# Attention units interleaved with an expert layer: transposes and outputs of a unit moved three and four places behind the next unit's scores

## The reference, cut to what matters

```python
# q, k, v: 4 batches x 8 heads x 576 positions x 64
q_d, k_d, v_d = (a.reshape(B, H, 144, 4, D).mean(axis=3) for a in (q, k, v))
out_up = np.repeat(softmax_attention(q_d, k_d, v_d), 4, axis=2)          # "down" part, 144 x 144
scores = np.where(abs(pos[:, None] - pos[None, :]) < 4, scale * q @ k.T, -1e9)
out_local = softmax(scores) @ v                                           # "local" part, a band of 7
x = (out_up + out_local).transpose(0, 2, 1, 3).reshape(2304, 512)
x = (silu(x @ w_gate) * (x @ w_val)) @ w_out                              # first layer, hidden 1536
h = x @ w_in                                                              # second layer, hidden 2048
out = (maximum(h, 0) + alpha * minimum(h, 0)) @ moe2_w_out
```

## The kernel before, in words

| after its scores | PE | ACT | DVE |
|---|---|---|---|
| 0 | scores, L933 and L923 | | mask, maxima, shift (L730 to L747) |
| 1 | | exponentials (L545, L538) | |
| 2 | | | sums and reciprocals (L753 to L760), after which POOL normalises (L484, L487) |
| 3 | | | average of v (L719) |
| 4 | | | flip of the local part (L768) |
| 5 | transposes of the down part (L964) | turn (L556, four copies), then copy of the transposes (L566) | average of the next unit's q and k (L708) |
| 7 | outputs, L980 and L993 | | `add_up` (L776, L779) |
| 8 | | `x_hi` (L570) | `x_lo` (L785) |

## Time and profile before

### The profile page before, as it was taken

The page is one execution under the profiler, slowest core; times in us unless marked ns, Lnnn a source line. Parts: engine busy times, 40 slices in busy tenths (PEclk is TensorE's granted clock), DMA queues, the critical chain, the costliest instruction groups (busy, mean ns, idle before and its releaser), DMA issues.

```text
span 958.6 us, 21368 instructions
## 1 busy us (share of the span) xinstructions
PE 938.9 (98%) x8808; PEld 883.4 (92%) x8808; DVE 520.7 (54%) x1072; ACT 290.7 (30%) x759; POOL 143.1 (15%) x166
## 2 busy tenths in 40 slices
PE   5999999999999999999999999999999999999998
PEld 3899999999999999999999999999999999999997
DVE  8787655656655656556543545444444444444443
ACT  5665332423334333323333522111111111111111
POOL 7875000000010010100005830000000000000000
PEclk7899999999999999999999999999999999999999
DMA  9752211312222213113006520010100100200000
GB/s 285 238 175 81 87 54 49 96 49 62 85 59 78 68 54 92 54 49 94 25 11 198 168 92 1 1 66 1 35 32 1 67 1 1 67 1 1 34 1 34
DMA packets 32142, 63.37 MB, mean 66 GB/s; under 512 B 3376, under 2 KB 14640, under 8 KB 32048
## 3 DMA queue, kind: packets, MB, share of 16 engines
q1 hardware_dynamic: 32048, 62.02, 20.5%
HBM read 52.57 MB, written 9.44 MB: 65 GB/s over the span
## 4 chain that ended last, share of the span: by engine, by line
PE 95%; DVE 2%; POOL 1%; issue 1%; ACT 1%; DMA 0%; DVEq 0%; SPq 0%
PE ps L1031 52%; PE ps L1076 21%; PE ps L1059 16%; PE ps L980 2%; PE ps L923 2%; PE ps L933 1%; POOL w_lo L468 1%; PE ps L993 1%; PE ps L964 1%; DMA qk<-qk 0%; PE ps L1040 0%; ACT turned_early L556 0%; POOL down_one L487 0%; DVE qk_d_early L708 0%; ACT down_one L538 0%
## 5 line engine op out<-in xcount | busy, mean ns | idle before, releaser
L1031 PE MATMUL ps<-x_hi,w_hi 128*128 128x288 f32 x765 | 231.6, 303 | 0.0
L1031 PE MATMUL ps<-x_lo,w_hi 128*128 128x288 f32 x765 | 225.8, 295 | 0.0
L1031 PE MATMUL ps<-x_hi,w_lo 128*128 128x288 f32 x765 | 225.2, 294 | 0.0
L626 ACT CAST h_hi<-hidden 128x288 fp32r<-128x288 f32 (+1 forms) x192 | 90.9, 473 | 397.5 <-DVE hidden L894 330.9
L862 DVE TENSOR_TENSOR h_lo<-hidden,h_hi 128x288 fp32r<-128x288 f32 (+1 forms) x192 | 114.5, 596 | 84.7 <-ACT h_hi L626 82.2
L1031 PEld LDWEIGHTS ps<-x_hi,w_hi 128*128 128x128 f32 x765 | 143.5, 188 | 2.9
L892 DVE TENSOR_SCALAR gated<-ps,alpha_sb 128x384 f32<-128x384 f32 x96 | 59.3, 618 | 159.6 <-PE ps L1031 159.6
L1031 PEld LDWEIGHTS ps<-x_hi,w_lo 128*128 128x128 f32 x765 | 143.9, 188 | 0.0
L1031 PEld LDWEIGHTS ps<-x_lo,w_hi 128*128 128x128 f32 x765 | 143.8, 188 | 0.0
L1059 PE MATMUL ps<-h_hi,w_hi 128*128 128x288 f32 x384 | 115.3, 300 | 0.7 <-DVE h_lo L862 0.7
L1076 PE MATMUL ps<-w_lo,h_hi 128*128 128x512 f32 x288 | 113.2, 393 | 0.0
(11 more groups left out here) (139 smaller groups left out, 1454.6 us busy)
## 6 DMA issues: line engine op xcount, KB each, us to landing
w_home<-w SPq DMA_DIRECT2D x68, 256.0 KB, 3.6
qk<-qk SPq DMA_DIRECT2D x30, 436.0 KB, 3.4
vsrc_one<-vsrc SPq DMA_DIRECT2D x58, 144.0 KB
vwin<-vwin SPq DMA_DIRECT2D x30, 192.0 KB, 2.4
y_t<-y_sb SPq DMA_DIRECT2D x8, 576.0 KB, 3.4
x_raw<-y_t SPq DMA_DIRECT2D x6, 768.0 KB, 5.8
out<-y_sb SPq DMA_DIRECT2D x5, 768.0 KB, 4.0
qk_early<-qk SPq DMA_DIRECT2D x2, 436.0 KB, 5.6
```

The source lines that it names most:

```text
L626: nc.scalar.copy(h_hi[r][:, 0:width], hidden[r][:, 0:width]).then_inc(h_hi_ready, 1)
L1031: mm = nc.tensor.matmul(out_ps, w[:, piece, 128 * k:128 * k + 128], x_parts[low][:, k, :], start=(k == 0 and n == 0), stop=(k == KC - 1 an ...
```

## The change

The places of the parts are now computed for each unit (class `Unit`, `schedule`), and every engine goes through the same list `WORK` by the place's number g, counted through the whole layer. The units are scored at places 1, 9, 18, 26 of a block. For the first three units of a block (`overlapped`: another unit of the same block is scored under 10 places later), transposes and the copy of them move to three places behind the *next* unit's scores, outputs and `add_up` to four, `x_hi` and `x_lo` to five. That is 11 and 12 places behind the unit's own scores (12 and 13 of the block for the first unit, 21 and 22, 29 and 30). The fourth unit of a block has no such follower: its transposes stay at 5 behind its scores (place 31), and its outputs stand at 6 (place 32) where they stood at 7. For all units the turn stays at 5 behind the scores and the flip at 4, and the average of the next unit's q and k moves from 5 to 1. On ACT, the copy of the transposes now stands before the turn where both fall on one place.

To keep this free of races `down` has two buffers, with one more memset on POOL, and PE waits for more semaphores ahead of scores (5 in place of 3) and of transposes (4, or 2 for the fourth unit, in place of 1). SP's list is written out without its loop; its order is the same, so `refill_vwin` of a unit now waits five places longer, and so does all behind it. The remaining edits (`SPANS`, `RING`, `x_at`) rename shapes that stay as they were.

```diff
-def scored_at(k):
-    return SLOT * k if k else 1
-def act_pieces(k):
-    return min(EARLY_PIECES + SLOT * k, P1)
+SCORED_IN = ((1, 9, 18, 26),) * (NB - 1)
+class Unit:
+    def __init__(self, q, block, place, following):
+        self.q, self.scored = q, PLACES * block + place
+        self.exponentials = self.next_averaged = self.scored + 1
+        self.summed = self.scored + 2
+        self.flipped = self.scored + 4
+        self.turned = self.flipped + 1
+        overlapped = following is not None and following - self.scored < 10
+        self.transposed = following + 3 if overlapped else self.flipped + 1
+        self.put_out = self.transposed + 1
+        self.overlapped = overlapped
+    for unit, last in zip(units, [None] + units):
+        unit.v_averaged = max(unit.flipped, last.put_out + 1 if last and last.overlapped else 0)
+        unit.outputs_before = PAIRS + sum(u.put_out < unit.scored for u in units)
+        unit.outputs_between = PAIRS + sum(u.put_out < unit.transposed for u in units)
...
 # POOL
+            nc.gpsimd.memset(down[1][1][:, :, :, CHUNK:TILE_K], 0.0).then_inc(gaps_zeroed, 1)
-            for k in range(PAIRS):
-                first, end = act_pieces(k), act_pieces(k + 1)
-                ahead = min(first + 4, end)
-                for j in range(first, ahead):
+            done = EARLY_PIECES
+            for unit in WORK:
+                ready = min(max(EARLY_PIECES + unit.scored + 3, done), P1)
+                for j in range(done, ready):
                     split_rest(j)
+                done = ready
+                normalise(unit.q, unit.q % PAIRS, 1)
 # ACT
                 if mode:
-                    act.wait_ge(down_turned, q)
+                    act.wait_ge(down_turned, q - 1)
...
+                for unit in WORK:
+                    a, k = divmod(unit.q, PAIRS)
+                    if g == unit.exponentials:
                         local_exponentials(a, k, 1)
                         down_exponentials(a, k, 1)
-                    if at == 5:
+                    if g == unit.transposed:
+                        copy_down_t(a, k, 1)
+                    if g == unit.turned:
                         turn_local(a, k, 1)
-                        copy_down_t(a, k, 1)
-                    if at == 8:
-                        split_x_hi(PAIRS * a + k, half, k, 1)
+                    if g == unit.put_out + 1:
+                        split_x_hi(a, k, 1)
 # DVE
+                for unit in WORK:
+                    a, k = divmod(unit.q, PAIRS)
+                    if g == unit.put_out:
+                        add_up(a, k, 1)
+                    if g == unit.scored:
+                        local_maxima(a, k, a % 2, 1)
                         down_maxima(a, k, 1)
+                    if g == unit.summed:
                         reciprocals(a, k, 1)
+                    if g == unit.flipped:
+                        flip_local(a, k, 1)
+                    if g == unit.put_out + 1:
+                        split_x_lo(a, k, 1)
+                    if g == unit.v_averaged:
                         average_v(a, k)
+                    if g == unit.next_averaged and unit.q + 1 < UNITS:
+                        average_qk(*divmod(unit.q + 1, PAIRS))
 # PE
                 if mode:
-                    pe.wait_ge(x_added, q)
+                    pe.wait_ge(x_added, outputs_before)
+                    pe.wait_ge(shifted, q)
+                    pe.wait_ge(down_ready, q)
...
-            def transpose_down(a, k, mode):
+            def transpose_down(a, k, mode, overlapped=False, outputs_before=0):
                 pe.wait_ge(down_normed, PAIRS * a + k + 1)
+                if mode:
+                    pe.wait_ge(x_added, outputs_before)
+                if overlapped:
+                    pe.wait_ge(shifted, PAIRS * a + k + 2)
+                    pe.wait_ge(down_ready, PAIRS * a + k + 2)
...
+                    if g == unit.scored:
+                        pair_scores(a, k, a % 2, 1, unit.outputs_before)
+                    if g == unit.transposed:
+                        transpose_down(a, k, 1, unit.overlapped, unit.outputs_between)
+                    if g == unit.put_out:
                         pair_outputs(a, k, 1)
```

More of the change, by code:

```diff
@@ L164, in build @@
         with ExitStack() as first_x:
-            x_hi = [sb(f"x_hi{r}", [128, KC, TB], F32R, where=first_x) for r in range(2)]
-            x_lo = [sb(f"x_lo{r}", [128, KC, TB], F32R, where=first_x) for r in range(2)]
+            x_hi = sb("x_hi", [128, KC, RING], F32R, where=first_x)
+            x_lo = sb("x_lo", [128, KC, RING], F32R, where=first_x)
         with ExitStack() as second_x:
@@ L178, in build @@
             down_t_alone = sb("down_t_alone", [CHUNK_ROWS, 2 * SEQ_D], where=alone)
[L179 to L183, removed]
+        gated = sb("gated", [128, WIDEST])
+        hidden = [sb(f"hidden{r}", [128, WIDEST]) for r in range(2)]
+        y_sb = sb("y_sb", [128, KC * WIDEST])
+        y1_sb = [y_sb[:, 0:KC * span].rearrange("p (k s) -> p k s", k=KC) for span in SPANS]
+        y2_sb = y_sb[:, 0:KC * TB2].rearrange("p (t f) -> p t f", t=TT)
         with ExitStack() as att:
@@ L194, in build @@
             local_one = sb("local_one", [128, 2 * TILES, GK], where=att)
-            down_one = sb("down_one", [HQ, 2, CHUNKS, TILE_K], where=att)
+            down_two = [sb(f"down{r}", [HQ, 2, CHUNKS, TILE_K], where=att) for r in range(2)]
             flipped_one = sb("flipped_one", [128, 2 * TILES, GK], where=att)
@@ L642, in split_loaded_x_hi, with first_block @@
                 nc.scalar.copy(x2_hi[half][:, k, :], x_raw[:, k, :]).then_inc(x_hi_ready, 1)
-            def first_block(j, half):
+            def first_block(j):
+                span = SPANS[j]
                 for p in range(PLACES):
@@ L1080, in outputs2, with first_block @@
                 mm.then_inc(bank_ready if last_block else h_used, 1)
-            def first_block(j, half):
+            def first_block(j):
+                x_here = [ring[:, :, HOMES[j]:HOMES[j] + SPANS[j]] for ring in (x_hi, x_lo)]
                 for p in range(PLACES):
@@ L1092, in first_block @@
                         pe.wait_ge(w_ready, 3 * c + 1)
-                        products(gate_ps, 3 * c, (x_hi[half], x_lo[half]), 0 if s else KC - 1).then_inc(gate_ready, 1)
+                        products(gate_ps[j], 3 * c, (x_here[0], x_here[1]), 0 if s else KC - 1).then_inc(gate_ready, 1)
                     if p % 3 == 1:
@@ L1096, in first_block @@
                         pe.wait_ge(w_ready, 3 * c + 2)
-                        products(val_ps, 3 * c + 1, (x_hi[half], x_lo[half])).then_inc(pre_ready, 1)
+                        products(val_ps[j], 3 * c + 1, (x_here[0], x_here[1])).then_inc(pre_ready, 1)
                     if p % 3 == 2 and s:
```

278 lines of the change are left out of this document (138 added, 140 removed).

## The result

The changed kernel takes 966.99 us in the median of 4 runs (966.59 to 967.75), the kernel before 961.16 us on the same chip (960.48 to 961.28): a ratio of 1.0064, with a 95% interval of 1.0053 to 1.0076. So the change costs 5.8 us. The forecast was slower, 964.8 us, range 961.3 to 968.5: direction and range hold, but the cost is 2.2 us above the forecast, and a large part of it stands where the prediction had put a gain. The profiled execution of the changed kernel took 966.77 us with a span of 965.0 us, 6.4 more than the span before.

What follows compares the result with a forecast made beforehand. PE was taken as the bound from block 1 on. Block 0's −2.4, seven waits' +5.95 and memset's +0.05 make +3.6 us on 960.35: 963.95, or 964.75 us in a median, range 961.3 to 968.5.

Steps and rivals of the forecast that it cites:

- the seven waits: Fourth unit of each block: PE's outputs wait for ACT's turn, 0.85 us each, 5.95 us in all.
- What bounds the kernel, and that nothing can be gained from block 1 on: PE is always busy from block 1 on, so moving transposes and outputs later gains nothing there.
- PE's added waits at nothing: Extra semaphore waits ahead of scores and transposes: taken at nothing; 0.1 us for each of 28 units would be 2.8.
- T + 2.76: Forecast start of the fourth unit's outputs, T being the start of its transposes; a wait of 0.78 us.
- Block 0 … −2.4: Block 0: moved transposes no longer wait for POOL three times, a gain of 2.4 us, bounds 1.8 to 2.9.
- about 0.5 us of the 0.9 turns into a wait for `h_lo`: Block 0, place 8: without the first POOL wait, PE waits about 0.5 us for DVE's low part, ended at 42.17.
- speaking for a smaller gain: Block 0: POOL contention also stretches DVE's moved `x_lo`, so the gain is nearer 1.8 than 2.9 us.
- The gain of the transposes in units 2 and 3: Block 0: transposes of units 1 to 3 come 10 us and more later, far beyond POOL's lateness, ending their waits.
- SP's later loads at nothing: Block 0: weight pieces behind the later `refill_vwin` hold ACT up to 4 us; PE cost nothing, at most 2 us once.
- The other 21 units: Transposes three places behind the next scores don't wait for exponentials, room near 1 us; rival with waits adds 4.2, 6%.
- POOL's memset: One more memset of 0.29 us, mostly covered by a wait for weights: 0.05 us taken, 0.25 at most.
- The clock rival: PE's new waits drop the clock to half, 8.5 us each, 60 in all, giving 1024 us; chance 2%.

Runs made afterwards that it cites:

- the run that takes them away: Changed kernel with the fourth unit's outputs two places behind its transposes instead of one: 962.03 us, ratio 1.0015.
- The run with gaps on POOL: Changed kernel where POOL, ahead of every third weight piece from 11 on in block 0, waits for DVE's low part: 961.21 us, ratio 1.0003.
- the repeated run: The changed kernel run again unchanged: 967.29 us, ratio 1.0068 to the kernel before.
- both repairs: Changed kernel with fourth unit's outputs one place later and POOL waiting for DVE's low parts in block 0: 956.48 us, ratio 0.9959; again 956.81.
- the old places: Changed kernel's code with scores, transposes, outputs, averages and turn placed as before the change: 957.1 us, ratio 0.9957; again 956.87.

## Why the prediction was right or wrong

Direction and range hold, but in part by luck. Block 0 came out 5.0 us above its term. Against that, the seven waits came out 1.65 below theirs, and the layout and the end of the kernel gave back 0.9 and 0.4 us that stood in no term. The start of the kernel added 0.85, which the change did not cause. Together that is about the 2.8 us by which the profiled execution lies above its forecast (966.77 against 963.95).

- **What bounds the kernel, and that nothing can be gained from block 1 on: right**, with one exception that lies outside of the places (the layout, below).
- **PE's added waits at nothing: right.** Places without a wait take 2.61 (scores), 1.88 (transposes) and 2.54 us (outputs) in both kernels.
- **The seven waits of the fourth unit's outputs: the mechanism right, the size too large.** 0.85 each was taken, 5.95 in all; they measure 0.61 each, 4.3 in all, and 5.3 by the run that takes them away. The link that was off is the 0.44 behind the copy. It was read from 223.93 and 224.37, but the instruction at 224.37 was itself waiting for `hidden`; behind a copy that is followed at once the next starts after 0.30 (92.47 to 92.77). The outputs start at T + 2.60 (94.24, with the transposes at 91.64), not T + 2.76, against T + 1.98 without a wait. The Trainium skill, page "ScalarE: Activation LUTs", section "What ACT_TABLE_LOAD costs", says that back-to-back ACTIVATEs overlap by about 93 ns; the trace agrees, with 0.41 to 0.42 us long and 0.30 to 0.33 apart.
- **"Block 0 … −2.4": wrong, and this is the step that failed.** Block 0, without its share of the seven waits, lost 2.6 instead, 5.0 off. The step said of the low part that "about 0.5 us of the 0.9 turns into a wait for `h_lo`". It took 1.71 for the low part's length and only moved its start. But 1.71 was that short because POOL paused at 41.85 until ACT's cast of 42.22 was done: this low part, too, did not get in at the first change of pieces (40.61), and ended 0.32 us behind the start of the pause. In the changed kernel POOL's run starts 1.07 later (40.39 against 39.32) and that cast 0.30 earlier (41.92), 1.37 nearer together, more than the pause was long. Of this, 0.43 is the copy of the transposes, which stood before the cast (41.79 to 42.22), and the rest is the average of v, which now stands behind the flip and no longer holds back flip and turn. (This split is read from the rows; the run with the first unit's old places brings back the copy and not the average of v, and with it a pause of 0.49 us.) So in the changed kernel POOL pauses nowhere, and the low part, which starts 0.94 later, gets through only when POOL is done: 5.50 us, a wait of 4.04, a place 4.96 us longer with the slow clock in it. The run with gaps on POOL shows that the missing pause did it, and the run with the first unit's old places shows the same at another point. What is not shown is why these low parts missed the changes between pieces at which others got in (last section): an unbroken run is needed for the long wait, but does not bring it about each time. The rule of the Trainium skill, page "SBUF — State Buffer", section "Who interferes with whom", on two SBUF inputs of DVE against GpSimd's reads, was named in the prediction as speaking for a smaller gain; it was worth 5 us, not 1.1, as DVE was held not for one instruction but for a run of five.
- **The gain of the transposes in units 2 and 3: right in size, wrong in cause.** The prediction gave it to the ten microseconds by which the transposes come later. One weight piece less ahead of POOL's normalising gives the same without any move (2.6 us). `act_pieces` and `ready` stood in the diff side by side: 4 pieces against `scored + 3`.
- **"The remaining edits … rename shapes that stay as they were": wrong**, and in no term of the sum. The layout of x gains 1.75 us by the medians, 1.0 of it seen in blocks 1 to 6 of its own profile, and 0.9 net in the same blocks of the changed kernel.
- **SP's later loads at nothing: right**, and as close as said. ACT stood for a weight piece once for 2.33 us (81.09), and no place of PE near it is longer.
- **The other 21 units, and POOL's memset: right**, no wait and 0.28 us.
- **The clock rival: it came, but small.** A stretch at half speed followed the 4 us wait, none the seven waits of 0.56. It costs about 1.4 us in the profile after and 2.6 in the repeated run, not 8.5 a time: the prediction priced it by the 17 us of the kernel's start, and the stretches here are 3.4 and 6.8 us.

Together: +4.3 (profile) to +5.3 (run) for the fourth unit, +6.1 for POOL's unbroken run and its clock, −2.6 for the piece, −1.75 for the layout, and −0.9 for the wait of the first unit's transposes, which only the move takes away: +5.2 to +6.2, and +5.8 was measured. That 0.9 is in the profiles (block 0 is 66.73 us with both repairs and 67.56 at the old places), but the other blocks give 0.2 of it back, the runs with gaps on POOL take 0.25 more outside of their span (2.02 against 1.77), and the medians are alike; whether anything is left of it stays open.

## What to carry to other kernels

Before taking a wait away, ask who lives in the idle time that it makes: here a DVE instruction with two SBUF inputs was let in by a pause of 1.07 us on POOL, and when an earlier cast on a third engine closed that pause it cost 5 us. A distance between two starts is a pitch only where the second instruction waited for nothing. And run "the rest of the diff" alone: two edits that looked like bookkeeping were worth some 4 us, and the moved places, at their best here, nothing that could be told.

## What the hardware showed that was not expected

A DVE subtraction of 128x288 in SBUF took 0.46 us alone, 0.60 beside a POOL that paused, and 5.50 and 5.20 us beside five and six POOL subtractions without a pause; it ended within 0.35 us of the last of them (46.90 against 46.60, 62.90 against 62.58). In both cases it got in between none of the pieces, though mostly DVE does. Over the fourteen traces DVE's `h_lo` and `x_lo` subtractions began 230 times in a POOL instruction that another followed at once. Of these, 217 ended 0.31 to 0.32 us behind the end of that first instruction, and where the next one was a weight piece it lasted about 1.5 us instead of about 1.3. Two got in at once. Eleven missed the first change, and each of them ended 0.31 to 0.32 us behind POOL's next stop: 1.70 to 1.85 us where POOL paused after one more piece, and 5.20 to 5.51 us in the five where it did not. Ten of the eleven are the same low part, the second of block 0. What makes it miss is open; how long the first piece still had to run (0.15 to 1.19 us) does not decide it, as others began at the same distance and got in.

And the spacing of fp32 product matmuls with 288 columns depends on how the moving operand is laid out: 131.7 to 131.8 ns for one half of the side-by-side tensor, 133.15 to 133.4 for the other, 133.0 for separate tensors. Which property of the address does it was not tried.
